# A recurrent attention and two feed-forward layers on one core: feed-forward weights loaded in smaller and earlier pieces, u transposed by four wide transposes, outputs in two halves, masked scores behind the inverses

## The reference

```python
for t in range(S):
    y[:, :, t] = np.einsum('bhd,bhde->bhe', rt, state)
    Sa = np.einsum('bhde,bhe->bhd', state, at)
    state_decay = state * wt[:, :, None, :] - np.einsum('bhd,bhe->bhde', Sa, bt)
    state = state_decay + np.einsum('bhd,bhe->bhde', vt, kt)
x = np.ascontiguousarray(attn_out.transpose(0, 2, 1, 3)).reshape(B * S, H * D)
# first layer: 320 -> 1024 -> 320
h = x @ w_in; e = np.exp(h - h_max); sm = e / (sum(e) + 1e-09); solu = h * sm
x = ((solu - mu) / np.sqrt(var + 1e-06) * g_ln) @ w_out
# second layer: 320 -> 2048 -> 320
h = x @ w_in; g = np.maximum(h, 0.0) + alpha * np.minimum(h, 0.0)
return g @ w_out
```

## Time and profile before

| | us |
|---|---|
| median of 3 runs | 1009.94 (1007.06 to 1019.16) |
| profiled execution, its own time | 1007.09 |
| its span in the trace | 1005.3 |
| attention, first PE work to the last output taken | to 431.7 |
| from there to the matmuls of chunk 1's first layer output | 431.7 to 499.13 |
| one feed-forward chunk after that | 45.85 |

### The profile page before, as it was taken

The page is one execution under the profiler, slowest core; times in us unless marked ns, Lnnn a source line. Parts: engine busy times, 40 slices in busy tenths (PEclk is TensorE's granted clock), DMA queues, the critical chain, the costliest instruction groups (busy, mean ns, idle before and its releaser), DMA issues.

```text
span 1005.3 us, 32828 instructions
## 1 busy us (share of the span) xinstructions
PE 914.6 (91%) x14016; PEld 864.9 (86%) x14016; DVE 653.6 (65%) x1135; ACT 438.1 (44%) x892; POOL 243.2 (24%) x453
## 2 busy tenths in 40 slices
PE   3379999998989989867799999999999999999997
PEld 3368989997888888757799999999999999999997
DVE  7966788885858665657556656475757566564744
ACT  4234454444435443335434435353635344353532
POOL 8676455674646550000000000000000000000000
PEclk9697999999979999999899999999999999999999
DMA  5726765567655444062110100000000000000000
GB/s 160 128 67 155 153 132 120 125 156 190 137 120 137 115 94 104 25 181 72 27 27 1 28 14 14 27 0 26 0 26 0 26 0 26 15 11 13 2 14 14
DMA packets 144004, 67.42 MB, mean 67 GB/s; under 512 B 120029, under 2 KB 129373, under 8 KB 143885
## 3 DMA queue, kind: packets, MB, share of 16 engines
q1 hardware_dynamic: 141772, 65.53, 26.9%
q10 hardware_dynamic: 2112, 0.13, 0.2%
HBM read 45.98 MB, written 19.66 MB: 65 GB/s over the span
## 4 chain that ended last, share of the span: by engine, by line
PE 61%; DVE 10%; POOL 9%; issue 6%; DMA 6%; SPq 5%; ACT 3%; DVEq 0%; ACTq 0%; POOLq 0%
PE acc L1091 5%; PE acc L1092 5%; PE acc L1093 5%; PE px L342 4%; PE bank L1091 3%; PE mid L1091 3%; SPq L232 3%; PE mid L1092 3%; PE bank L1093 3%; PE bank L1092 3%; PE mid L1093 3%; POOL s_x L818 3%; POOL s_t L816 3%; PE pq L404 2%; PE bank L1124 2%
## 5 line engine op out<-in xcount | busy, mean ns | idle before, releaser
L1352 POOL TENSOR_TENSOR stats<-stats 128x1 f32<-128x1 f32 x24 | 13.2, 549 | 558.0 <-DVE stats L1414 558.0
L1439 DVE SCALAR_TENSOR_TENSOR stage<-mid,slopes 128x512 f32<-128x512 f32 x96 | 66.4, 691 | 109.8 <-ACT slopes L1278 109.8
L1091 PE MATMUL acc<-wo_h,act_h 128*128 128x320 f32 x384 | 122.3, 319 | 16.4 <-DVE act_l L1366 15.8
L1274 ACT ACTIVATE stage<-mid 128x512 f32<-128x512 f32 x96 | 57.0, 594 | 159.6 <-PE mid L1162 159.6
L1092 PE MATMUL acc<-wo_h,act_l 128*128 128x320 f32 x384 | 119.0, 310 | 0.0
L1093 PE MATMUL acc<-wo_l,act_h 128*128 128x320 f32 x384 | 118.6, 309 | 0.0
L1091 PE MATMUL mid<-zT_h,w_h 128*128 128x256 f32 x384 | 107.9, 281 | 0.0
L1092 PE MATMUL mid<-zT_h,w_l 128*128 128x256 f32 x384 | 107.6, 280 | 0.0
L1093 PE MATMUL mid<-zT_l,w_h 128*128 128x256 f32 x384 | 107.4, 280 | 0.0
L795 POOL TENSOR_TENSOR al<-al,prod 40x512 f32<-40x512 f32 x48 | 67.2, 1400 | 104.6 <-DMA al<-a_features_first 92.3
L1091 PEld LDWEIGHTS acc<-wo_h,act_h 128*128 128x128 f32 x384 | 72.6, 189 | 21.3 <-issue 19.2
(11 more groups left out here) (152 smaller groups left out, 2368.5 us busy)
## 6 DMA issues: line engine op xcount, KB each, us to landing
wkb<-wkb_features_first SPq DMA_DIRECT2D x46, 242.5 KB
rvu<-rv_features_first SPq DMA_DIRECT2D x48, 160.0 KB
l_scr<-lb SPq DMA_DIRECT2D x24, 256.0 KB, 4.3
x_scr<-x SPq DMA_DIRECT2D x24, 256.0 KB, 3.7
al<-a_features_first SPq DMA_DIRECT2D x48, 80.0 KB
sv<-v_time_first SPq DMA_DIRECT2D x48, 80.0 KB, 4.8
out<-y_sb SPq DMA_DIRECT2D x12, 320.0 KB, 2.3
d_scr<-s_x SPq DMA_DIRECT2D x12, 256.0 KB, 2.3
```

The costliest lines, as they stand in the source:

```text
L1091: pe.matmul(o, left[0], right[0], start=start, stop=False)
L1274: act.activation(neg[q % 2][:], mid[q % 2][:], ACT.Relu, scale=-1.0).then_inc(neg_ready, 1)
L1439: dve.scalar_tensor_tensor(out=act_f[q % 2][:], in0=mid[q % 2][:], scalar=0.0, in1=slope[q % 2][:], op0=ALU.max, op1=ALU.add).then_inc(act ...
```

## The change

- `w_in` is loaded in twelve DMAs of 128 KB, one at each n from 4 to 15, in place of three of 512 KB; the three small constants come at n = 2 and not at n = 7.
- Of the second layer's weights pieces 3 and 2 are issued at n = 21 and 22, chunk 1's x and pieces 0 and 1 at n = 23, pieces 8, 10, 11 and 9 right after the last output is saved; pieces from 8 on go round four buffers. `BESIDE` is 10: ten pieces are split before `take_z(0)`, and chunk 1's x before all of them.
- `solve_u` makes u alone, now for all 24 chunks. ACT writes minus u into `nu` (zeros between the heads), and `turn_u` turns it by four 128x128 transposes; `take_uT` takes them by four copies in place of two.
- `outputs(n)` is cut in two: heads 0 to 3 at the end of step n, heads 4 to 7 in step n + 1. `turn_kb(n+6)` moves from the end of step n to behind `turn_u` of step n + 1.
- DVE does `take_horner` 2 and 3 each before a half of `mask_ka`; ACT does `spread_state` before `copy_l(n+6, 0)` and `take_rhs` before `copy_l(n+6, 1)`.

```diff
@@ tensor @@
         def solve_u(m):
             pe.wait_ge(x_taken, 4 * m + 4)
             pe.wait_ge(rhs_ready, m + 1)
-            if m + 2 < NG:
-                for h in range(NH):
-                    for half in range(2):
-                        ins = pe.matmul(pr[HR[half], h * HD:(h + 1) * HD], hh[HR[half], h], rhs[HR[half], h],
-                                        start=True, stop=True)
-                ins.then_inc(u_done, 1)
-            wait(pe, sn_ready, m - 1)
             for h in range(NH):
                 for half in range(2):
-                    ins = pe.matmul(pu[ER[half], h * T:(h + 1) * T], rhs[HR[half], h], hh[HR[half], h],
+                    ins = pe.matmul(pr[HR[half], h * HD:(h + 1) * HD], hh[HR[half], h], rhs[HR[half], h],
                                     start=True, stop=True)
+            ins.then_inc(u_done, 1)
+
+        def turn_u(m):
+            pe.wait_ge(nu_ready, m + 1)
+            wait(pe, sn_ready, m - 1)
+            for j in range(NH // 2):
+                ins = pe.transpose(pu[:, j * P:(j + 1) * P], nu[:, 2 * j:2 * j + 2].rearrange("p a b -> p (a b)"), ident)
             ins.then_inc(uT_done, 1)
...
-        def outputs(m):
+        def outputs(m, part):
-            for h in range(NH):
+            for h in range(part * 4, part * 4 + 4):
...
             solve_u(n)
             if nxt:
                 horner(n + 1, 0)
+            turn_u(n)
             beside(pe, n, "early")
+            if 0 < n and n + AHEAD - 1 < NG:
+                turn_kb(n + AHEAD - 1)
             if n > 0:
-                outputs(n - 1)
+                outputs(n - 1, 1)
             read_out(n)
...
                 horner(n + 1, 3)
                 right_side(n + 1)
-            if front:
-                turn_kb(n + AHEAD)
+            outputs(n, 0)
@@ vector @@
+            if nxt:
+                take_horner(n + 1, 2)
             if front:
                 mask_ka(n + AHEAD, 0)
             if nxt:
-                take_horner(n + 1, 2)
+                take_horner(n + 1, 3)
             if front:
                 mask_ka(n + AHEAD, 1)
-            if nxt:
-                take_horner(n + 1, 3)
@@ scalar @@
         def take_u(m):
             act.wait_ge(u_done, m + 1)
-            for half in range(2):
-                act.mul(sv[m % 3][HR[half], half], heads(pr, NH, HD)[HR[half]], -1.0).then_inc(u_ready, 1)
+            act.mul(nu[:, :, 0:HD], heads(pr, NH, HD), -1.0).then_inc(nu_ready, 1)
+            if m + 2 < NG:
+                for half in range(2):
+                    act.mul(sv[m % 3][HR[half], half], heads(pr, NH, HD)[HR[half]], -1.0).then_inc(u_ready, 1)
...
-                act.mul(vuT[m % 3][ER[half], half], heads(pu, NH, T)[ER[half]], -1.0).then_inc(uT_ready, 1)
+                dst = vuT[m % 3][ER[half], half].rearrange("p (j e) t -> p e j t", e=2)
+                for e in range(2):
+                    act.copy(dst[:, e], src[ER[e], :, half]).then_inc(uT_ready, 1)
@@ feed-forward, sync_beside @@
-        elif n in (8, 9, 10):
-            sp.dma_start(w1_raw[:, n - 8], wts["w_in"][:, n - 8]).then_inc(w1_loaded, 16)
-        elif n == 12:
+        if 4 <= n < 16:
+            k, cols = (n - 4) // 4, slice((n - 4) % 4 * 256, (n - 4) % 4 * 256 + 256)
+            sp.dma_start(w1_raw[:, k, cols], wts["w_in"][:, k, cols]).then_inc(w1_loaded, 16)
+        if n == 12:
...
+        elif n == 21:
+            sp.wait_ge(att["rhs_done"], 21)
+            load_piece(sp, 3)
+        elif n == 22:
+            sp.wait_ge(att["horner_taken"], 4 * (NG - 2))
+            load_piece(sp, 2)
         elif n == NG - 1:
+            sp.wait_ge(att["horner_done"], 4 * (NG - 1) + 1)
+            load_x(sp, 1, second_x)
             sp.wait_ge(early_low, len(first))
+            load_piece(sp, 0)
+            load_piece(sp, 1)
@@ feed-forward, sync @@
         for saved in att["y_saved"]:
             sp.wait_ge(saved, NG // 2 * 16)
-        load_piece(2)
-        load_x(sp, 1, x_in[1])
-        for n in range(4, len(pieces)):
-            load_piece(n)
+        load_piece(sp, 8)
+        load_piece(sp, 10)
+        load_piece(sp, 11)
+        sp.wait_ge(xT_low, 2)
+        load_piece(sp, 9)
+        for n in range(4, EARLY):
+            load_piece(sp, n)
+        for n in range(12, len(pieces)):
+            load_piece(sp, n)
+        sp.wait_ge(low_ready, len(pieces))
@@ feed-forward, scalar prologue (vector's likewise) @@
             take_n(0, 1)
+            take_x(act, 1, second_x)
             for saved in att["y_saved"]:
                 act.wait_ge(saved, NG // 2 * 16)
-            for n in range(6):
+            for n in range(BESIDE):
                 split_high(n)
-            take_x(act, 1, x_in[1])
-            split_high(6)
-            split_high(7)
             take_z(0)
```

More of the change, by code:

```diff
@@ L350, in right_side @@
             wait(pe, sv_ready, 2 * (m - 1))
+            wait(pe, nu_ready, m)
             wait(pe, u_ready, 2 * min(m, NG - 2))
@@ L431, in outputs @@
                     ins = pe.matmul(o, sn[m % 3][:, h], r_bd[m % 3][:, half, h], start=False, stop=True)
-            ins.then_inc(y_done, 1)
+            if part == 1:
+                ins.then_inc(y_done, 1)
         def prologue():
@@ L483, in tensor @@
             step(n)
-        outputs(NG - 1)
+        outputs(NG - 1, 1)
     def vector(dve, beside):
@@ L555, in take_horner @@
             elif stage == 1:
-                wait(dve, uT_done, m)
+                wait(dve, u_done, m)
                 dve.tensor_tensor(hh[:], pair[:, 1, g], p, ALU.subtract).then_inc(x_taken, 1)
@@ L734, in prologue @@
             act.wait_ge(a_bd_set, 1)
-            act.copy(pu[:], a_bd[:, 0].rearrange("p h t -> p (h t)")).then_inc(psum_set, 1)
             act.copy(py[:], a_bd[:, 0].rearrange("p h t -> p (h t)")).then_inc(psum_set, 1)
-            act.wait_ge(psum_set, 2)
+            act.wait_ge(psum_set, 1)
             spread_a(0)
@@ L755, in step @@
             front = n + AHEAD < NG
+            take_u(n)
+            take_uT(n)
             if 0 < n and n + AHEAD - 1 < NG:
                 take_kbn(n + AHEAD - 1)
-            if n + 2 < NG:
-                take_u(n)
-            take_uT(n)
             if n == 0:
@@ L777, in step @@
             if front:
+                copy_l(n + AHEAD, 0)
+            if n + 1 < NG:
+                take_rhs(n + 1)
+            if front:
                 copy_l(n + AHEAD, 1)
             beside(act, n, "late")
-            if n + 1 < NG:
-                take_rhs(n + 1)
         prologue()
@@ L943, in feed_forward @@
     raw_loaded = [sem(f"raw_loaded{i}") for i in range(4)]
-    late_loaded = [sem(f"late_loaded{i}") for i in range(2)]
+    late_loaded = [sem(f"late_loaded{i}") for i in range(4)]
     high_ready, low_ready = sem("weights_high"), sem("weights_low")
@@ L971, in feed_forward @@
     staging = [stage[0], stage[1], slopes, stage2]
-    late = [late_stage, y_sb[:].rearrange("p a b -> p (a b)")]
-    STAGES, EARLY = len(staging), 8
-    late_home = {n: 0 if n in w2_piece.values() else 1 for n in range(EARLY, len(pieces))}
+    late = [y_sb[:].rearrange("p a b -> p (a b)"), late_stage] + [z[:].rearrange("p k t -> p (k t)") for z in x_in]
+    STAGES, EARLY, BESIDE = len(staging), 8, 10
+    second_x = late_stage[:, 0:KT * 2 * P].rearrange("p (k t) -> p k t", k=KT)
+    late_home = {n: (n - EARLY) % len(late) for n in range(EARLY, len(pieces))}
     late_before = {n: [m for m in late_home if m < n and late_home[m] == late_home[n]] for n in late_home}
@@ L1323, in step @@
                 rectify(c, q)
-                if isinstance(c, int) and c == 0 and q < (len(pieces) - EARLY) // 2:
-                    split_high(EARLY + 2 * q)
-                    split_high(EARLY + 2 * q + 1)
+                if isinstance(c, int) and c == 0 and q < (len(pieces) - BESIDE) // 2:
+                    split_high(BESIDE + 2 * q)
+                    split_high(BESIDE + 2 * q + 1)
                 if nxt and q == 1:
@@ L1490, in prologue @@
             low_n(0, 1)
-            for n in range(6):
+            low_x(dve, 1, second_x)
+            for n in range(BESIDE):
                 split_low(n)
-            low_x(dve, 1, x_in[1])
-            split_low(6)
-            split_low(7)
             low_z(0)
@@ L1502, in step @@
                 split(c, q)
-                if isinstance(c, int) and c == 0 and q < (len(pieces) - EARLY) // 2:
-                    split_low(EARLY + 2 * q)
-                    split_low(EARLY + 2 * q + 1)
+                if isinstance(c, int) and c == 0 and q < (len(pieces) - BESIDE) // 2:
+                    split_low(BESIDE + 2 * q)
+                    split_low(BESIDE + 2 * q + 1)
                 if nxt and q == 0:
```

45 lines of the change are left out of this document (22 added, 23 removed).

## The result

The changed kernel takes 1004.8 us (median of 17 runs, 1000.46 to 1012.9), the kernel before in the same rounds 1010.0 (17 runs, 1007.06 to 1020.86): ratio 0.993, interval 0.9906 to 0.9956. The forecast was 986.4. The direction was right, but only a quarter of the 20.7 us came, and the time lies outside the range of 974 to 1000. The profiled execution took 1006.4 us with a span of 1004.5; before these were 1007.1 and 1005.3. The two traces are thus less than 1 us apart where the medians are 5.2 apart: they show where time went and came, and not the last few microseconds of the result.

What follows compares the result with a forecast made beforehand. Attention was taken as bound by the SP and POOL loop (15.0 us a step), close to PE's 14.5, with waits for weights behind it. 1007.1 profiled minus 13.8 (attention) minus 6.9 (behind it) gave 986.4 us; range 974 to 1000.

Steps and rivals of the forecast that it cites:

- PE's step: Attention step on PE that waits for nothing: 0.4 us saved of 14.5, the new wait for `nu` covered by `horner(n+1, 0)`.
- The loop's turn: Attention's loop through SP and POOL: a turn per pair of steps takes 30.0 us, plus 2.4 in all for small loads.
- PE's own slack then takes most of it: Attention: if PE halts inside a matmul group again, its slack of 0.9 us a step absorbs most of the halt.
- The loop sets the pace: Attention: pairs come every 30.0 us, PE waits about 2 us in two steps; `horner(20, 0)` starts 12.3 us earlier.
- The last steps: Last four steps of attention: 1.5 us more won, including 1.1 lost in the last step.
- Behind attention: From attention's end to chunk 1's output: 6.9 us gained because waits for late weight loads go.
- the wait for z: Behind attention: PE idles 7 us before chunk 0's second layer, in place of 5.46 us waiting for chunk 1's x.
- order waits: Behind attention: about 3.2 us left because splits and chunk 1's softmax stand ahead of a pair's products on DVE and ACT.
- Rival 1: Attention: the loop does not bind, as its transfers run faster with emptier DMA queues; 976 us, chance 0.13.
- Rival 2: PE's stalls stay and the last ten splits are late, 5 us more in each place; 996 us, chance 0.25.
- Rival 3: Early weights help nowhere, and `l_write` behind a later copy of L stretches the loop; 1002 us, chance 0.08.
- Rival 4: Attention: DVE's chain becomes the bound, with POOL and DVE stretching each other; 1030 us, chance 0.04.

Runs made afterwards that it cites:

- run 1: Changed kernel with `turn_kb` and ACT's copies of kbn back at their old places: 1004.16 us, ratio 0.992 to the kernel before.
- run 11: run 5 with `turn_kb` and `take_kbn` back at their old places: 996.17 us, ratio 0.984 to the kernel before.
- run 12: Changed kernel with less load traffic from group 5 on (`w` columns of wkb not reloaded, only 64 columns of rv): 1002.09 us, ratio 0.988 to the kernel before.
- run 4: Changed kernel with SP's order in odd steps altered, `load_a` ahead of `d_read` and `l_read` in its middle: 996.83 us, ratio 0.984 to the kernel before.
- run 3: Kernel before with only the `w_in` loads spread (twelve of 128 KB, constants at n = 2): 1014.02 us, ratio 1.0004 to the kernel before.
- run 6: Changed kernel with `load_a` moved behind `l_read` and `load_wkb` in SP's order: 1035.59 us, ratio 1.025 to the kernel before.
- run 8: Attention of the changed kernel with the feed-forward of the kernel before: 1011.01 us, ratio 1.000 to the kernel before.
- run 9: Kernel before with only SP's order altered from step 3 on, `load_a` ahead of `d_read`, `l_read` in its middle: 1016.93 us, ratio 1.006 to the kernel before.
- run 7: Attention of the kernel before with the feed-forward of the changed kernel: 1000.83 us, ratio 0.988 to the kernel before.
- run 2: Changed kernel with `first_high` moved from the end of steps 19 and 21 to the middle of 20 and 22: 998.76 us, ratio 0.986 to the kernel before.
- run 10: run 5 with the attention code of the kernel before: 1003.34 us, ratio 0.992 to the kernel before.
- run 5: Changed kernel with `load_a` ahead of `d_read`, `l_read` in its middle (from step 3), and `first_high` amid steps 20 and 22: 988.37 us, ratio 0.975 to the kernel before.

## Why the prediction failed

**PE's step: more than forecast, and worth nothing.** 0.7 us saved for 0.4; the rest is the wait for `hh` ahead of the last `horner` (3.9 us in 14 steps before, none now), which DVE's new order of `take_horner` and `mask_ka` takes away and which the prediction did not count. The four transposes took 0.50 as forecast, the four copies 1.5 (0.368 each), DVE had room. Costing `turn_kb`'s move at nothing was right with the loop as it is (run 1), and would not be with a shorter one (run 11).

**The loop's turn: the step that failed.** `horner(20, 0)` was to come 12.3 us earlier than 365.74 and came 2.9 earlier. I took 30.0 from two turns and put the rest of the average down to large loads and constants. The parts of a turn, means of the same seven turns, worked out from the starts in each trace:

| | d_write to load_a | to scale_a | to solve | to d_write | turn |
|---|---|---|---|---|---|
| turn from 129.84, before | 8.9 | 3.1 | 2.8 | 15.4 | 30.15 |
| before | 9.8 | 3.6 | 2.7 | 15.2 | 31.3 |
| changed | 10.2 | 3.4 | 2.9 | 14.8 | 31.2 |
| run 12 | 9.0 | 3.9 | 2.5 | 15.7 | 31.0 |
| run 4 | 5.6 | 4.6 | 4.7 | 15.1 | 30.0 |

The term was 7 x 30.0 + 2.4, and 7 x 31.2 came: 6.2 us of the 9.4 that are missing. The large loads were not the cause of the difference (run 3). The loop is not a clock of its own: `l_write` waits for copies of L, which wait for `scores`, which wait for `a_bd` from POOL. A halt of PE lengthens the turn in which it falls: behind the halts at 148.12 and 161.05 SP waited 4.6 us for the copy of L, and `load_a` of the turn to 194.77 went out 14.3 us behind its `d_write`. So "PE's own slack then takes most of it" was wrong: the overlap that the prediction counted on isn't there. That the halts alone make 31.2 of 30.0 is not shown. In run 12 they are gone and `load_a` goes out after 9.0 us, as in the quiet turn, but `solve` takes 0.9 more and the turn stays at 31.0. `horner(20, 0)` then started at 362.81, 13.4 us behind its `d_write` where I had 11.2 (2.2 more of the 9.4; the last 1.0 was there at the start, 130.80 for 129.8), and with no wait on `dd`: there it was PE that was late.

**"The loop sets the pace" was half of the truth.** It does in the changed kernel (runs 1, 4, 6, 12). In the kernel before PE's chain stood as near: a pair of clean steps is 28.9 us, plus its halts. Shortening either alone brings nothing (runs 8, 9: ratios 1.000 and 1.006). With the new feed-forward, and without the waits for `nu` that spoil run 8, the four cases are: neither 0.988 (run 7), PE's step alone 0.986 (run 2), the loop alone 0.992 (run 10, with `first_high` moved as well), both 0.975 (run 5). So one alone moves the time by -2 to +4 us, and both together by -13. The change shortened one of two.

**The last steps: 1.5 forecast, a loss of 7.2 came.** Steps 20 and 22 lost 5.4 us to `nu` behind `first_high`, the 6.0 of run 2: the second step that failed. I had written that `horner(n+1, 0)` covers the copy, from durations, and not looked at what stands ahead of it on ACT. The last step took 1.2 longer, as forecast (1.1), and steps 18 and 19 0.3 each.

**Behind attention: right.** 6.9 forecast, 7.2 measured up to chunk 1's output, and ratio 0.988 for that part alone (its interval reaches from 6 to 19 us); the 1.5 us at the end of the last chunk were not forecast; the wait for z 6.9 (forecast 7), the rest of order waits 2.4 (3.2).

Rival 1 (a loop that doesn't bind) has its sign in the trace, clean steps under 14.8 us with hardly a wait on `dd`, and is refuted all the same by runs 4, 6 and 12. Rival 2 had the mechanism that won, halts that stay, with its splits late by less than it said (chunk 0's second layer starts 19.8 us behind the output layer's start for 18.2): it gave 996. Its sign, `take_z(0)` over 20 us behind attention's end, tells nothing, since the kernel before had 20.6 there. Rival 3 was wrong in its first half; its `l_write` behind a later copy is in the trace (164.64). Its 1002 lies nearest to the measured time, but by luck, since the early weights did help. Rival 4 did not come. Still open: why `solve` takes 14.8 us in one trace and 15.7 in another, whether run 9 is slower or merely equal, and what keeps the turns at 31 us once the halts are gone.

## What to carry to other kernels

Where two chains have nearly the same length and wait for each other, the edit of one shows no gain, in either order; test them together before dropping either. Take the length of a loop from the mean of all its turns, and explain the long ones by their own waits before removing them from the sum. For each new instruction on an engine look up what stands ahead of it in that engine's order, and what that waits for.

## What the runs showed of the hardware

- PE halts in the middle of a group of matmuls, or at its start, with no semaphore late: six times for 0.5 to 2.5 us between 95 and 350 us in the changed kernel. Each ends 1.4 to 1.7 us behind the end of a 16 KB packet of the queue "instruction" (146.64 and 148.12; 159.54 and 161.05; 187.35 and 188.88); such packets come every 5 us on average, so this is hardly chance; that PE waits there for its instructions is the likely reading of it, not a measured one. With 111 GB/s from 95 to 350 us in place of 137 (DMA share 0.50 for 0.59) three halts are left, 0.8 us for 9.3 (run 12).
- Behind the wait of 2.70 us in step 20 PE runs at 1.2 GHz for 3.4 us; the step takes 20.4 us for 17.1. From 95 to 350 us the granted clock is 0.93 in run 6, where PE waits 39 us, and 0.97 in the changed kernel, where it waits 21.
- POOL starts on a 160 KB load of A 6.0 us after its issue when 485 KB of another load are issued just ahead of it, and 3.4 to 3.5 when none are (run 6, and the changed kernel).
